# Scoring two query tiles of head 2 from the split buffer in three 64-row products

## The reference

```python
q_rot, k_rot = (rotate(q), rotate(k))
scores = scale * np.matmul(q_rot, k_rot.transpose(0, 1, 3, 2))
scores = scores - np.max(scores, axis=-1, keepdims=True)
attn = np.exp(scores)
attn = attn / (np.sum(attn, axis=-1, keepdims=True) + 1e-09)
return np.matmul(attn, v).astype(np.float32)
...
xt = x.transpose(0, 2, 1)
h = xt @ U @ V
u = x + h.transpose(0, 2, 1)
ch = np.maximum(u @ w_ch1, 0.0) @ w_ch2
return (u + ch).astype(np.float32)
```

## Time and profile before

| | |
|---|---|
| time, median of 3 runs | 743.56 us (743.52 to 744.1) |
| profiled execution | 743.78 us, of which the span of the profile is 742.0 us |
| busy share of the span | PE 96%, PEld 86%, DVE 55%, ACT 59%, POOL 62% |
| granted TensorE clock, mean | 0.998 |
| instructions | 12350 |

### The profile page before, as it was taken

One profiled execution on the slowest core, in us unless ns is written; L12 is line 12 of the kernel. 1 busy time (PEld: TensorE's weight loads), 2 busy tenths in 40 slices (PEclk: granted clock), 3 DMA queues, 4 the chain that ended last, 5 costly groups with the idle time before them and its releaser, 6 DMA issues.

```text
span 742.0 us, 12350 instructions
## 1 busy us (share of the span) xinstructions
PE 711.1 (96%) x4314; PEld 640.6 (86%) x4314; DVE 406.1 (55%) x677; ACT 441.0 (59%) x951; POOL 463.5 (62%) x335
## 2 busy tenths in 40 slices
PE   9899986999999989999999999899999999999997
PEld 4788875999997879999999988898999888999986
DVE  5899997655557764444454566676565441112111
ACT  2888876767766655556656665676666334333331
POOL 3999865585867654764956867638333255656563
PEclk9999999999999999999999999999999999999999
DMA  7966684537474447357284373462622253434341
GB/s 203 270 192 178 184 257 124 175 105 215 145 215 123 145 147 236 114 156 234 86 232 167 105 218 130 150 185 75 164 73 102 100 187 126 165 127 171 127 171 72
DMA packets 73757, 117.84 MB, mean 159 GB/s; under 512 B 27040, under 2 KB 27168, under 8 KB 71904
## 3 DMA queue, kind: packets, MB, share of 16 engines
q1 hardware_dynamic: 73472, 116.68, 51.9%
q10 hardware_dynamic: 224, 0.36, 0.2%
HBM read 80.15 MB, written 9.44 MB: 121 GB/s over the span
## 4 chain that ended last, share of the span: by engine, by line
PE 74%; DVE 9%; ACT 8%; issue 6%; POOL 2%; DMA 1%; POOLq 0%; SPq 0%; ACTq 0%; DVEq 0%
PE ps L1151 25%; PE ps L1167 23%; PE ps L1050 7%; PE ps L1064 7%; PE ps L1085 5%; DVE negmax L877 3%; ACT prob L720 2%; PE ps L1019 2%; ACT pth L731 1%; PE ps L1077 1%; ACT low L737 1%; ACT w2h L784 1%; DMA stack<-raw 1%; PE ps L1133 1%; DVE hs L961 1%
## 5 line engine op out<-in xcount | busy, mean ns | idle before, releaser
L655 POOL TENSOR_TENSOR w2l<-w2u,w2h 128x512 fp32r<-128x512 f32 x96 | 123.9, 1291 | 223.0 <-ACT w2h L784 223.0
L978 DVE SCALAR_TENSOR_TENSOR htl<-ps,hth 128x384 fp32r<-128x384 f32 x96 | 53.5, 558 | 180.1 <-ACT hth L791 179.5
L877 DVE TENSOR_REDUCE negmax<-ps 128x1 f32<-128x576 f32 (+1 forms) x160 | 120.2, 751 | 51.1 <-PE ps L1050 44.6
L731 ACT ACTIVATE pth<-ps 128x512 fp32r<-128x512 f32 (+1 forms) x156 | 87.7, 567 | 82.5 <-PE ps L1085 81.2
L720 ACT ACTIVATE prob<-ps,negmax 128x576 f32<-128x576 f32 (+1 forms) x160 | 118.0, 738 | 28.3 <-DVE negmax L877 28.1
L1151 PE MATMUL ps<-ub,w1h 128*128 128x384 f32 x384 | 133.2, 347 | 1.1 <-DVE htl L978 0.6
L1151 PE MATMUL ps<-ub,w1l 128*128 128x384 f32 x384 | 129.8, 338 | 0.0
L1151 PE MATMUL ps<-utl,w1h 128*128 128x384 f32 x384 | 129.6, 337 | 0.0
L649 POOL TENSOR_TENSOR w1l<-w1u,w1h 128x512 fp32r<-128x512 f32 x96 | 124.2, 1294 | 5.4 <-ACT w1h L780 5.4
L791 ACT ACTIVATE hth<-ps 128x384 fp32r<-128x384 f32 x96 | 47.0, 490 | 131.8 <-PE ps L1151 131.4
L1050 PE MATMUL ps<-stack 128*128 128x288 f32 x620 | 112.0, 302 | 8.2 <-ACT prob L720 7.5
(11 more groups left out here) (84 smaller groups left out, 1133.6 us busy)
## 6 DMA issues: line engine op xcount, KB each, us to landing
w1u<-in_w SPq DMA_DIRECT2D x96, 256.0 KB, 2.6
w2u<-in_w SPq DMA_DIRECT2D x96, 256.0 KB, 2.7
stack<-raw SPq DMA_DIRECT2D x60, 288.0 KB, 4.5
raw<-in_qk SPq DMA_DIRECT2D x14, 1152.0 KB, 5.2
stack<-raw SPq DMA_DIRECT2D x60, 144.0 KB, 4.0
v2u<-in_v SPq DMA_DIRECT2D x16, 320.0 KB, 4.1
ubu<-scratch_u SPq DMA_DIRECT2D x18, 256.0 KB, 3.7
out<-ubu SPq DMA_DIRECT2D x18, 256.0 KB, 2.5
```

The costliest lines, as they stand in the source:

```text
L655: nc.gpsimd.tensor_tensor(w2l[:, at], w2u[:, at], w2h[:, at], ALU.subtract).then_inc(w2_lo, 1)
L731: nc.scalar.activation(pt_of(g)[0][rows, keys, queries], source, ACT.Copy).then_inc(pt_hi, 1)
L877: nc.vector.tensor_reduce(negmax[0:WT[t], t:t + 1], scores_of(n, WT[t]), AX.XY, ALU.max, negate=True).then_inc(maxed, 1)
```

## The change

The first two tiles of head 2 (tiles 10 and 11) are scored like head 0's, with three products of 64 rows out of the split buffer of round 1. The stack of head 2 is still made, and tiles 12 to 14 use it; PE's wait for it moves from tile 10 to tile 12. At tile 10 PE waits instead for the high and low parts of round 1. Round 1's parts are now written and read under the name `first`, and its low parts are written as fp32r. Since PE now reads round 1's buffer until tile 11, `load(3)` gets one more wait.

```diff
+DIRECT = 2
...
     def split_of(r):
-        return raw if r else first[:, :, :, :, :].bitcast(F32)
+        return raw if r >= 2 else first[:, :, :, :, :].bitcast(F32)
...
                         sp.wait_ge(scored, NT)
+                if r == 1:
+                    sp.wait_ge(scored, 2 * NT + DIRECT)
...
                 pool.wait_ge(qk_hi[which], r + 1)
-                nc.gpsimd.tensor_tensor(x, x, xs, ALU.subtract).then_inc(lo_split[which], 1)
+                if r == 1:
+                    xs, rest = first[:, 1, 1, which].bitcast(F32), first[:, 1, 0, which]
+                else:
+                    rest = x
+                nc.gpsimd.tensor_tensor(rest, x, xs, ALU.subtract).then_inc(lo_split[which], 1)
...
-                rounded = raw[:, r % 2, 1, which].bitcast(F32R) if r else first[:, 0, 1, which]
+                rounded = first[:, r, 1, which] if r < 2 else raw[:, r % 2, 1, which].bitcast(F32R)
...
-                if t == 0 and g:
+                if t == (DIRECT if g == 2 else 0) and g:
                     pe.wait_ge(stacked[g % HEADS_STACKED], stacks_done(g))
...
-                if g == 0:
+                if g == 0 or g == 2 and t < DIRECT:
+                    r = g // 2
+                    if g and t == 0:
+                        pe.wait_ge(qk_hi[0], r + 1)
+                        pe.wait_ge(qk_hi[1], r + 1)
                     for q, k in ((1, 1), (1, 0), (0, 1)):
-                        if n == 0 and q + k == 1:
-                            pe.wait_ge(lo_split[1 if q else 0], 1)
+                        if t == 0 and q + k == 1:
+                            pe.wait_ge(lo_split[1 if q else 0], r + 1)
                         for c in range(2):
                             mm = nc.tensor.matmul(ps[0:WT[t], at + c * BANK:at + c * BANK + CH],
-                                                  first[0:D, 0, q, 0, QO[t]:QO[t] + WT[t]],
-                                                  first[0:D, 0, k, 1, CH * c:CH * c + CH],
+                                                  first[0:D, r, q, 0, QO[t]:QO[t] + WT[t]],
+                                                  first[0:D, r, k, 1, CH * c:CH * c + CH],
                                                   start=(q + k == 2), stop=(q == 0))
```

## The result

The changed kernel is slower: a median of 747.04 us (743.48 to 749.4, 13 runs) beside 744.01 us for the kernel before (742.71 to 746.85, 13 runs), a ratio of 1.0029 with a 95% interval of 1.0015 to 1.0042. I had forecast 743.3 us and no measurable change. The profiled execution took 747.44 us, with a span of 745.6 us and a mean granted clock of 0.991 (before: 743.78, 742.0 and 0.998).

The account below looks back on a forecast made before the run. PE was taken to bound the kernel, with DVE and ACT as often on the chain from 20 to 125 us. Profiled 743.78 - 0.29 = 743.49, against the median 743.27, said as 743.3 us; range 742.4 to 744.4.

Parts of the forecast that it names:

- What bounds the kernel: PE overall, DVE and ACT as often from 20 to 125 us; tile 10 waits 0.88 us for head 2's stack.
- What costs nothing: New name, fp32r low parts, tile 10's new waits and the later `load(3)`: zero, at most a few tenths on SPq.
- 33.5: Sign of being wrong: round 3's load issued later than 33.5 us.
- the cover: At `load(3)`: issued at 33.42 us, tile 11's scores complete by 33.08, so 0.34 us of cover for its added wait.
- The 64-row tiles, tiles 10 to 12: Each costs PE 0.45 us more plus 0.16 to 0.19 per passage; DVE's maxima at 31.18, 33.08 and 35.00 us.
- Gain there: 0.55 us: At tile 10: scores start at 30.12 instead of 30.90, so DVE's maximum starts at 31.18 instead of 31.73.
- the sum's 0.29 us: Gain left at tile 11, maximum at 33.08 instead of 33.37, taken off the profiled execution's 743.78 us.
- PE is the one that pays: Rival: time follows PE's work, decided at tile 12, 0 to 0.21 us later, 743.6 to 743.8 us; chance 0.13.
- Does it reach the end: Claimed the 0.29 us shift passes through head 6, the later rounds and PE's fixed order from 130 us.
- The slack of about 0.6 us at head 6: Head 6's k transfer there by about 64.6 us, PE scoring at 65.19, so the 0.29 us shift fits.
- The shift is swallowed later: Rival: POOL's stretch, a stack or a weight load holds a later tile, 743.6 us; chance 0.13.
- another low stretch appears: Rival: one more stretch at 1.2 GHz, or the one near 126 to 130 us grows, 745.0 to 745.3 us; chance 0.05.

Follow-up runs that it names:

- `DIRECT = 0`: The changed kernel with all its edits except the direct tiles, the stack awaited at tile 10 as before: 744.04 us, ratio 0.9999 to the kernel before.
- the delayed kernels: The kernel before with extra 288-column matmuls, result overwritten, ahead of tiles 10 and 11 (2 and 2, or 5 and 2): 745.54 and 750.14 us.

## Why the prediction was wrong, point by point

- **What bounds the kernel.** Right as a place: tile 10's wait in the profile lay on the chain. Wrong as a description of the kernel. "PE loads weights for tile 10 after 0.88 us of idle time that ended with this transfer" was a property of that one execution. Six of eight profiles of the same order of work up to there do not have it, and I had not asked how firm a wait on a transfer is.
- **What costs nothing.** Right within what can be measured. `DIRECT = 0` measured 0.9999 (0.9986 to 1.0012). The low parts took 1.41 and 1.40 us as fp32r. `load(3)` went out at 34.23 us, later than the 33.5 that I had named as a sign of being wrong, but a transfer released it, and in the repeated profile of before it left at 33.98. With five direct tiles the cover is gone and the queue behind it pays, as the text had it.
- **The 64-row tiles, tiles 10 to 12.** Right against the profile used (31.10, 32.98 and 34.91 for 31.18, 33.08 and 35.00). That they are this close is in part luck: the execution was 0.18 us early ahead of tile 10, and counted from there each came about 0.1 us later than forecast. The rule of the Trainium skill, TensorEngine Tiling (Array Packing), Key Properties, that a change of mode drains TensorE, agrees with the 0.16 to 0.17 us of idle weight loads at each passage.
- **The failed step** is the "Gain there: 0.55 us" of tile 10, from which the sum's 0.29 us follows: "It starts at 29.53 + 0.59 = 30.12 instead of 30.90". 30.90 was the late case. From the usual 29.82 the same working gives a loss, and the profiles show it: tile 10's and tile 11's maxima 0.45 and 0.69 us later, tile 12's 0.72 and tile 45's about 0.6. The medians at a clock of 1.0 say 1.2 us for both tiles (0.3 to 1.4). This alone does not give 747.04; the other failed term is the clock, below.
- **The rival "PE is the one that pays"** is the mechanism that held, but at tile 10 and not at tile 12, where I had put its deciding point, and so at 0.6 to 1.2 us and not at 0 to 0.2.
- **Does it reach the end.** Right in the main for a delay: 0.5 us at tile 10 became 0.7 at the end, a figure that is itself uncertain by half a microsecond. The slack of about 0.6 us at head 6 was a good estimate, and it tells for the other case: a schedule whose stack came in time is 0.9 us ahead of the stalled one, more than the slack, and is held there by 0.21 to 0.41 us. The rival "The shift is swallowed later" is true of that part.
- **The clock.** The rival "another low stretch appears" had a chance of 0.05 and a price of 1.7 us each, a stretch that lowers the mean clock by 0.0023. The price was on the high side: from a clock of 0.998 to 0.989 the kernel before loses 3.5 us (743.19 to 746.69), 0.9 us for 0.0023, and the changed kernel 3.8 us from 0.995 to 0.989, 1.4 for 0.0023 (estimates from these medians). The chance was wrong twice: I took the low stretch of the earlier trace rows for a fixed part of the schedule, though every execution has its own number of them (the kernel before's clock runs from 0.989 to 0.998), and I thought that an unchanged idle time near 122 us left the rest unchanged. The changed kernel's mean clock is lower by 0.0022, worth roughly half of its 2.4 us; the forecast had this at nothing.

What stays open: why the clock falls more often in the changed kernel. Its work in the places concerned is the same, somewhat shifted. Whether it is the shift alone or something of the 64-row tiles was not shown, since the delayed kernels moved by other amounts than the changed one; a plain delay of 0.7 us at tile 11 without extra matmuls elsewhere would be the test.

## What to carry to other kernels

A stall in one profiled execution that ends on a transfer is a sample. Before pricing its removal, see what the same instruction does in a second execution; if the transfer is sometimes in time, the removal is worth a fraction of the stall, while the work that replaces it is paid every time. Where PE has idle times of a few microseconds and a mean clock below 1.0, compare executions at equal clock, and try useless matmuls in the longest gap before moving work about: here that was worth 0.19% (0.06 to 0.31), and the change that took away a wait cost 0.29%. A wait added to a transfer's issue costs nothing only as long as what stands behind it in the queue is not due.

## What the runs showed of the hardware

- The number of low-clock stretches differs from execution to execution of one kernel: the mean granted clock of the kernel before took values from 0.989 to 0.998 over 170 executions, with medians of 743.2 us at 0.998 (34 executions) and 746.7 at 0.989 (7).
- The same four stack transfers, issued at nearly the same time (the first k part at 24.27 and at 24.09 us), landed in time for tile 10 in one execution and 0.9 us late in another.
- Matmuls whose result nobody reads keep the clock up: with PE kept busy in five places its mean was 0.9996, beside 0.9936 for the kernel before on that chip.
- At a granted clock of 1.0 the executions of one kernel still spread from 742.73 to 744.88 us.
